# Attention, MLP and routed experts on one core: the next up product ahead, the token turn later, low parts in halves

## The reference

```python
scores = scale * q @ k.T + bias                  # B=2, H=8, S=768, head_dim=64
a = softmax(where(is_global | is_local, scores, -1e9)); x = a @ v    # 8 global keys, window of 96
h = x @ w_in                                     # 1536 tokens, 512 -> 2048
x = (maximum(h, 0) + alpha * minimum(h, 0)) @ w_out          # 2048 -> 512
logits = x @ w_gate + modality_bias[modality_id]             # 8 experts
e_idx = argmax(logits); gate_w = softmax(logits)[e_idx]
for e in range(E):                               # 512 -> 1024 -> 512
    out[mask_e] = gate_w[mask_e] * (maximum(x[mask_e] @ w1[e], 0) @ w2[e])
```

## Time and profile before

| | |
|---|---|
| Median of three runs | 594.56 us (593.52 to 595.53) |
| The profiled execution | 593.55 us, of which the span from first to last instruction is 591.8 |
| TensorE busy | 577.8 us, 98% |
| DVE, ACT, POOL busy | 331.5, 187.1, 122.0 us |
| Attention | to about 105 us |
| The four MLP groups | to about 385.5 us |
| Routing beside tile 0 | to about 407.4 us |
| Fourteen looped tiles | to the end, 12.6 to 12.8 us each, the first 13.5 |
| TensorE's granted clock | 0.997 of full speed |

### The profile page before, as it was taken

The page is one execution under the profiler, slowest core; times in us unless marked ns, Lnnn a source line. Parts: engine busy times, 40 slices in busy tenths (PEclk is TensorE's granted clock), DMA queues, the critical chain, the costliest instruction groups (busy, mean ns, idle before and its releaser), DMA issues.

```text
span 591.8 us, 10667 instructions
## 1 busy us (share of the span) xinstructions
PE 577.8 (98%) x3305; PEld 485.5 (82%) x3306; DVE 331.5 (56%) x852; ACT 187.1 (32%) x435; POOL 122.0 (21%) x187
## 2 busy tenths in 40 slices
PE   8999999999999999999999999999999999999995
PEld 4777778888989999899988999877778787877874
DVE  5877888787544465444554568775221289721211
ACT  4888887442010000100001004131221377521121
POOL 4444544997000000000000000101211113211110
PEclk9999999999999999999999999999999999999998
DMA  7976642562010000100001008014511169211110
GB/s 151 198 151 101 148 122 62 154 190 85 1 54 1 0 1 1 53 0 0 0 0 54 1 0 285 18 54 157 218 53 35 35 189 358 95 53 36 35 53 16
DMA packets 74544, 47.63 MB, mean 80 GB/s; under 512 B 52751, under 2 KB 60943, under 8 KB 74512
## 3 DMA queue, kind: packets, MB, share of 16 engines
q1 hardware_dynamic: 70288, 39.50, 23.9%
q0 software_dynamic: 2480, 7.34, 3.8%
q10 hardware_dynamic: 1744, 0.39, 0.3%
HBM read 40.93 MB, written 7.08 MB: 81 GB/s over the span
## 4 chain that ended last, share of the span: by engine, by line
PE 90%; DVE 5%; DMA 2%; issue 2%; ACT 1%; DVEq 0%
PE wide L1247 12%; PE wide L1249 11%; PE wide L1248 11%; PE wide L1235 9%; PE bank L1247 9%; PE bank L1249 9%; PE bank L1248 9%; PE bank L1407 4%; PE wide L1482 4%; PE bank L1507 4%; PE bank L1410 2%; DMA xg<-x_scratch,src_i 2%; PE wide L1346 2%; PE wide L1242 1%; PE bank L1495 1%
## 5 line engine op out<-in xcount | busy, mean ns | idle before, releaser
L865 DVE TENSOR_SCALAR h_act<-bank,alpha_sb 128x384 f32<-128x384 f32 x62 | 38.3, 617 | 106.3 <-PE bank L1249 106.3
L1247 PE MATMUL bank<-x_hl,wts 128*128 (+1 forms) x248 | 85.3, 344 | 0.0
L1249 PE MATMUL bank<-x_hl,wts 128*128 (+1 forms) x248 | 83.6, 337 | 0.0
L1248 PE MATMUL bank<-x_hl,wts 128*128 (+1 forms) x248 | 83.3, 336 | 0.0
L1247 PE MATMUL wide<-wts,h_h 128*128 128x512 f32 x192 | 75.7, 394 | 2.3 <-DVE h_l L868 2.3
L1249 PE MATMUL wide<-wts,h_l 128*128 128x512 f32 x192 | 75.9, 395 | 0.0
L1248 PE MATMUL wide<-wts,h_h 128*128 128x512 f32 x192 | 75.7, 394 | 0.0
L1124 DVE TENSOR_TENSOR hg_l<-wide,hg_h 128x256 fp32r<-128x256 f32 (+1 forms) x45 | 21.7, 510 | 59.8 <-ACT hg_h L605 59.5
L1247 PE MATMUL wide<-wts,hg_h 128*128 (+1 forms) x120 | 51.3, 427 | 0.2
L756 POOL DMA_INDIRECT xg<-x_scratch,source x1 | 1.9, 1920 | 226.9 <-DVE source L1021 226.9
L1247 PEld LDWEIGHTS bank<-x_hl,wts 128*128 128x128 f32 x248 | 46.6, 188 | 1.7
(11 more groups left out here) (217 smaller groups left out, 1040.0 us busy)
## 6 DMA issues: line engine op xcount, KB each, us to landing
stage<-in_moe_w SPq DMA_DIRECT2D x32, 512.0 KB, 7.5
ring<-in_moe_w_in SPq DMA_DIRECT2D x16, 256.0 KB, 2.9
ring<-in_moe_w_out SPq DMA_DIRECT2D x16, 256.0 KB, 2.9
v_raw<-in_v SPq DMA_DIRECT2D x16, 192.0 KB, 2.8
x_scratch<-x2row SPq DMA_DIRECT2D x4, 768.0 KB, 3.8
k_raw<-in_k SPq DMA_DIRECT2D x14, 192.0 KB, 3.3
q_raw<-in_q SPq DMA_DIRECT2D x14, 192.0 KB, 3.9
v_win<-in_v SPq DMA_DIRECT2D x16, 96.0 KB, 2.6
```

Source lines behind the costliest of these rows:

```text
L865: link(ts(h, acc, 0.0, alpha_sb[:, j:j + 1], ALU.min, ALU.mult))
L1247: pe.matmul(acc, lhs[0], rhs[0], start=start, stop=False)
L1248: pe.matmul(acc, lhs[0], rhs[1], start=False, stop=False)
L1249: return pe.matmul(acc, lhs[1], rhs[0], start=False, stop=stop)
```

## The change

Three things are changed.

- TensorE, MLP: in every group but the last, up(0) of the next group is issued ahead of this group's down(15); the next group then begins with up(1).
- Low parts: DVE makes the first hidden half's low part in two operations of 256 columns, so that `hg_low` rises by four per tile. All waits are renumbered.
- Looped tile: `turn_x(t + 1)` moves from ahead of down chunk 0 to behind down chunk 1, and `turn_h(t, 1)` from behind chunk 1 to behind chunk 0. ACT and DVE do the second hidden half ahead of the next tokens accordingly. Tile 0 keeps its order on TensorE.

```diff
@@ ACT, tile @@
                 hidden_row(t, 1)
+                hidden_high(t, 1)
                 gathered_high(t + 1)
-                hidden_high(t, 1)
@@ DVE, hidden_low @@
-                for c0, c1 in (((4, 6), (6, 8)) if u else ((0, 4),)):
+                for c0, c1 in (((4, 6), (6, 8)) if u else ((0, 2), (2, 4))):
@@ DVE, tile @@
                 split(1, 2)
+                hidden_low(t, 1)
                 gathered_low(t + 1)
-                hidden_low(t, 1)
@@ TensorE, group @@
-                    if not first:
-                        nxt(0)
                     for j in range(FC):
                         if j + 1 < FC and not (first and j < 2 * AHEAD - 1):
                             nxt(j + 1)
+                        if j == FC - 1 and not last:
+                            up(g + 1, 0, 0, banks[0])
                         if j == 0:
                             pe.wait_ge(x2_copied, 2 * g + 2)
                         down(j)
@@ TensorE, tile @@
                     up_part(t, o, 1, range(2, 4))
+                    pe.wait_ge(y_copied, t + 1)
+                    pe.wait_ge(hg_low, 4 * t + 1)
+                    down_part(t, o, [0])
+                    turn_h(t, 1)
+                    down_part(t, o, [1])
                     turn_x(t + 1)
-                    pe.wait_ge(y_copied, t + 1)
-                    pe.wait_ge(hg_low, 3 * t + 1)
-                    down_part(t, o, range(2))
-                    turn_h(t, 1)
-                    down_part(t, o, range(2, 4))
-                    pe.wait_ge(hg_low, 3 * t + 2)
+                    pe.wait_ge(hg_low, 4 * t + 2)
+                    down_part(t, o, [2, 3])
+                    pe.wait_ge(hg_low, 4 * t + 3)
                     down_part(t, o, range(4, 6))
-                    pe.wait_ge(hg_low, 3 * t + 3)
+                    pe.wait_ge(hg_low, 4 * t + 4)
                     down_part(t, o, range(6, 8))
```

More of the change, by code:

```diff
@@ L1445, in after_attention @@
                 pe.wait_ge(y_copied, 1)
-                pe.wait_ge(hg_low, 1)
+                pe.wait_ge(hg_low, 2)
                 down_part(0, 1, range(2))
@@ L1458, in after_attention @@
                 down_part(0, 1, range(2, 4))
-                pe.wait_ge(hg_low, 2)
+                pe.wait_ge(hg_low, 3)
                 down_part(0, 1, range(4, 6))
-                pe.wait_ge(hg_low, 3)
+                pe.wait_ge(hg_low, 4)
                 pe.wait_ge(tiles_known, 1)
```

## The result

The change makes the kernel faster by 0.7%: the ratio to before is 0.9928, 95% interval 0.9914 to 0.9942. The medians of ten runs each are 588.92 us (588.37 to 590.91) and 593.26 us (592.14 to 595.53). The forecast of 592.1 (590.0 to 594.4) was too high, and the result lies under its range. The gain is 4.3 us where 2.4 were forecast. That is 1.9 of the 3.2 us between 592.1 and 588.9; the other 1.3 are the base, since the three runs shown before the prediction have their median 1.3 us above that of the ten.

What follows compares the result with a forecast made beforehand. TensorE, busy 577.8 of 591.8 us, was taken as the bound. Terms: -3.01 + 0.2 + 0.07 + 0.84 + 0.2 - 0.71 = -2.4 us, against a median of 594.56 giving 592.1; 8-in-10 range 590.0 to 594.4.

Steps and rivals of the forecast that it cites:

- The MLP boundaries: Dense MLP, three group boundaries: six TensorE stops at down(15) and the next down(0) go, -3.01 us; +0.2 for late copies.
- late copies: Dense MLP boundaries: down(0) may wait for ACT to copy out the accumulators it overwrites, +0.2 us for three boundaries together.
- down(0) behind the up product: Looped tile: down(0), now right after the last up matmul, waits for its low operation, +0.19 us per tile.
- The turn behind relu: Looped tile: the second hidden half's turn, now one chunk after the up product, waits for ACT's relu, +0.05 us per tile.
- The stop at down(4): Steady looped tile: TensorE's wait at down(4) for the second hidden half's low part goes, -0.18 us per tile.
- The first looped tile: Its turn of the next tokens comes 1.8 us later, which covers the wait for the gather, -0.71 us.
- The low part in halves: First hidden half's low part on DVE takes two operations, hidden in looped tiles but on tile 0's path, +0.07 us once.
- The three tiles with a new expert: DVE comes about 0.1 us later there because a weight split is in front, +0.2 us with what follows.
- The step that failed: Steady expert tile: claimed one stop inside, at down(4), where 0.18 us is lost.
- The first rival: Looped tiles gain: TensorE returns from register waits as fast as from constant ones, -2.0 in place of +0.84, 589.3 us; chance 0.15.
- The rule that I set against the trace: Engine instructions can queue during sequencer control work; spoke for quick returns from waits, but the trace's 0.65 us did not bear it out.

Runs made afterwards that it cites:

- the tile part alone: Kernel before with the looped tile's new order and the first half's low part in two operations, MLP as before: 591.82 us, ratio 0.9967.
- the halves alone: Kernel before with only the first hidden half's low part split into two operations and waits renumbered, order as before: 595.15 us, ratio 1.0025.
- the 27 of before beside the first experiments: A count, not a run's number: 27 runs of the unchanged kernel before, made beside follow-up runs; 22 had a mean clock above 0.994, median 593.2 us.

## Why the prediction was wrong

The mechanisms that I priced were there, most of them nearly at their price. One gain was left out. That the kernel became faster, as forecast, rests on the MLP part; for the tile part alone the sum had +0.4, and -1.5 was measured.

- **The MLP boundaries,** -3.01 + 0.2: right. -2.8 by the times, -2.99 by the start of the first looped tile. The 0.2 for late copies was not needed.
- **down(0) behind the up product,** +0.19 per tile: measured +0.20. **The turn behind relu,** +0.05: +0.02. **The stop at down(4),** -0.18: gone.
- **The first looped tile,** -0.71: 13.49 to 12.66 is -0.83, of which 0.12 is what every tile gained. Right in that trace, though the stop is not in every execution.
- **The low part in halves,** +0.07 once: not seen by itself. That it costs nothing where it is hidden was too simple, as the run with the halves alone showed.
- **The three tiles with a new expert,** +0.2: too small. They changed by -0.11, +0.11 and +0.23 us; beside the -0.12 of the others that is +0.6. In the last two down(0) loses 0.57 and 0.61 us where a steady tile loses 0.20: DVE came some 0.4 us later and not 0.1. The timeline shows the weight split in front of the low part in the second of them:

```profile
486.15 1.23 DVE L996 TENSOR_TENSOR wts<-stage,wts 128x1024 f32 x1 [0.37 <-issue]
486.29 0.59 ACT L605 CAST hg_h<-wide 128x512 fp32r<-128x512 f32 x1
...
487.29 0.75 DVE L1124 TENSOR_TENSOR hg_l<-wide,hg_h 128x256 fp32r<-128x256 f32 x2
...
487.94 0.19 PEld L1247 LDWEIGHTS wide<-wts,hg_h 128*128 128x128 f32 x1 [0.73 <-issue]
```

The high part is there at 486.88, but DVE's split runs from 486.15 to 487.38, and the load comes at 487.94, 0.65 after the low operation's start.

- **The step that failed** is the sentence that a steady tile "has one stop inside, at down(4)". It went on to price the tile's new order by that stop and the two new ones, and took the start of the tile as given. The sum knew that the low part would end earlier, and put the worth of this for the next tile's start at nothing. The start had lost 0.14 us too, and the runs show that this loss goes with how late the tile's last low operation ends: 2.7 us before the next tile in the kernel before, 3.7 us in the changed one, where nothing is lost. Thirteen passages make that 1.8 us, nearly all of the 1.9 that the gain was short by. With it the tile part is -1.4 and not +0.4; -1.5 was measured. The terms that were off beside it (+0.4 for the new experts, -0.4 for the turn behind relu, +0.1 for down(0), -0.2 for the copies) nearly cancel, which is luck.
- **The first rival** (the tiles gain, 589.3) came nearest in its number, by luck and not by its mechanism: TensorE comes back from the wait in down(0) as late as forecast, 0.66 us after the operation's start.
- The rule that I set against the trace (the Trainium skill, Advanced Engine Details and Errata, Sequencer Loop: other engine instructions can be read and queued while the sequencer does control work) fits another place than the one where I looked. It does not shorten the return from a wait that blocks, which 0.66 us shows again. It would explain the tile's start, which costs nothing when the last low operation ends 3.2 us or more ahead, and 0.5 us or more at 1.95; no trace shows the queueing itself.

What is shown is that the loss at a tile's start comes and goes with how late the tile's last low operation is ready, even where TensorE's array does not stop for it. Low operation and TensorE meet in the wait on `hg_low` alone, so the wait is the likely link. In the kernel before, the low operation for which down(4) stops and the last one end within 0.4 us of each other, and which of the two waits makes its 0.14 us is not told apart. That the time goes into the loop's branch, the value loads and the register arithmetic at the start is the likely reading of idleness that no engine's release ends; the profile shows them too coarsely to add them up, and it was not tried to take them out one by one.

## What to carry to other kernels

In this kernel a wait whose release comes late could cost twice: where it stands, and at the next turn of the loop. The second part showed up as idle time with no releaser, away from the wait, and it was there although the wait itself stopped nothing. So when an order is changed, list the small stops that end in "issue" too, and ask how far ahead of them the last thing waited for was ready: here 3.2 us was enough and 2.8 was not. Here the better order was a smaller edit than the one made: a filler that needs nothing new (the token turn) directly behind the up product, and the turn of the second half one chunk earlier, leaves no stop inside a steady tile and gives 585.2 us.

## What the runs showed of the hardware

TensorE's granted clock fell for some microseconds in the routing stretch in 4 of the 10 runs of the changed kernel, and in 5 of the 27 of before beside the first experiments. The windows of the changed kernel's profile around it (span of the window and its length, then busy time with instruction counts of PE, PEld, DVE, ACT and POOL, then the granted clock, DMA share and GB/s):

```profile
383.00:388.00 5.00, 5.00 (x39) 4.55 (x38) 3.66 (x4) 2.20 (x5) 0.00 (x0) 1.00 0.43 161
389.00:395.00 6.00, 6.00 (x17) 4.45 (x17) 2.95 (x17) 1.29 (x3) 0.00 (x0) 0.50 0.00 0
395.50:400.00 4.50, 4.11 (x27) 3.44 (x26) 4.16 (x18) 1.18 (x2) 0.00 (x0) 1.00 0.00 0
```

From 389 to 395 us the clock is 0.50 of full, its lower level of 1.2 GHz, and a 512-column matmul starts every 0.43 us instead of 0.23. Before it fell TensorE had done turns and products of 8 columns (L1346) between products of 512, and it was not idle: 5.00 of 5.00 us are busy. In the trace of before the same stretch is at full clock. At the lower clock the kernels take 1.1 to 2.9 us more (588.6 and 590.6 for the changed one, 593.2 and 595.9 for before). No edit was aimed at this, and whether the change makes it more frequent can't be said from so few runs.
